# Constant waits in TensorE's loop, group work in single pieces, and weight loads put among tiles 3 to 11, in a fused attention, routing and expert kernel

## The reference

```python
scores = scale * np.matmul(q, k.transpose(0, 1, 3, 2))        # B = H = 8, S = 576, 64 per head
ret = scores * Dmat                                           # Dmat = gamma[h] ** (i - j) for i >= j, else 0
x = np.matmul(ret, v)                                         # then 4608 tokens x 512
logits = x @ phi                                              # 512 x 32 slots
d = exp(logits - logits.max(0)); d /= d.sum(0) + 1e-9         # over tokens
slot_input = d.T @ x                                          # 32 x 512
for e in range(8): slot_out[e] = np.maximum(slot_input[e] @ w1[e], 0) @ w2[e]
c = exp(logits - logits.max(1)); c /= c.sum(1) + 1e-9         # over slots
y = c @ slot_out
out = (((y @ fw1) * (y @ fw2)) @ w3) @ w_out
```

## Time and profile before

| | us |
|---|---|
| median of 3 runs (lowest, highest) | 422.67 (421.44, 427.01) |
| the profiled execution | 421.35 |
| its span, first to last instruction | 419.6 |
| TensorE busy | 359.9 (86% of the span), granted clock 0.972 |
| VectorE, GpSimd, ScalarE busy | 170.1, 162.5, 120.7 |
| DMA | 104.77 MB, 250 GB/s on average |

### The profile page before, as it was taken

How to read it: one execution, slowest core, us unless ns; L and a number is a source line. 1 busy time by engine, 2 the same in 40 slices (tenths; PEclk the granted TensorE clock), 3 DMA queues, 4 the chain that set the end, 5 groups by cost and what they waited for, 6 DMA issues and landing times. The chain is left out here.

```text
span 419.6 us, 16276 instructions
## 1 busy us (share of the span) xinstructions
PE 359.9 (86%) x7123; PEld 276.3 (66%) x7123; DVE 170.1 (41%) x353; ACT 120.7 (29%) x248; POOL 162.5 (39%) x155
## 2 busy tenths in 40 slices
PE   2568878878887788764999999989999999999996
PEld 1557766767576667652566655547878888888885
DVE  1334545655474466415400310069993223323220
ACT  1011121211121122122232523053264444454532
POOL 1520221122202122025435655139894555555530
PEclk9996999999898999986999999999999999999999
DMA  8557788888688779625799999705633555666322
GB/s 253 211 195 261 290 319 334 311 316 326 250 312 307 309 273 357 250 94 202 315 419 418 419 419 416 300 2 124 204 113 124 198 178 197 222 213 216 125 100 100
DMA packets 25914, 104.77 MB, mean 250 GB/s; under 512 B 2660, under 2 KB 5284, under 8 KB 16164
## 3 DMA queue, kind: packets, MB, share of 16 engines
q1 hardware_dynamic: 25892, 104.47, 66.8%
HBM read 94.14 MB, written 10.32 MB: 249 GB/s over the span
## 5 line engine op out<-in xcount | busy, mean ns | idle before, releaser
L546 POOL TENSOR_TENSOR pkg_sb<-pkg_sb,const_sb 128x512 f32<-128x512 f32 x36 | 37.7, 1048 | 128.6 <-DMA pkg_sb<-in_tiles 128.6
L602 POOL TENSOR_TENSOR feat<-c_sb 128x512 f32<-128x512 f32 x45 | 56.9, 1275 | 46.2 <-PE psum L999 44.3
L665 PE MATMUL psum<-weights_t,pkg_sb 64*64 64x64 f32 x1152 | 33.6, 232 | 31.8 <-issue 13.8
L999 PE MATMUL psum<-m_hi,feat_hi 128*128 128x512 f32 x144 | 56.1, 390 | 0.3 <-DVE m_lo L1453 0.3
L999 PE MATMUL psum<-m_lo,feat_hi 128*128 128x512 f32 x144 | 56.0, 389 | 0.0
L999 PE MATMUL psum<-m_hi,feat_lo 128*128 128x512 f32 x144 | 56.0, 389 | 0.0
L419 DVE TENSOR_TENSOR feat_lo<-feat,feat_hi 128x512 fp32r<-128x512 f32 x34 | 27.2, 800 | 62.2 <-ACT feat_hi L1140 61.0
L1015 ACT COPY x_nat<-psum 128x512 f32<-128x512 f32 x36 | 21.1, 585 | 108.2 <-PE psum L673 108.2
L1239 DVE TENSOR_TENSOR x_t<-psum,x_decay 128x512 f32<-128x512 f32 x36 | 24.9, 692 | 62.2 <-PE psum L665 62.2
L665 PEld LDWEIGHTS psum<-weights_t,pkg_sb 64*64 64x64 f32 x1152 | 26.3, 142 | 35.6 <-issue 35.5
L576 POOL TENSOR_TENSOR w_lo<-fold_raw,w_hi 128x512 fp32r<-128x512 f32 x16 | 21.1, 1321 | 51.8 <-ACT wo_hi L1073 51.7
(11 more groups left out here) (125 smaller groups left out, 565.0 us busy)
## 6 DMA issues: line engine op xcount, KB each, us to landing
pkg_sb<-in_tiles SPq DMA_DIRECT2D x34, 1024.0 KB, 4.9
unit_a<-in_units SPq DMA_DIRECT2D x16, 1024.0 KB, 12.2
c_sb<-c_rows SPq DMA_DIRECT2D x45, 256.0 KB
unit_x<-in_units SPq DMA_DIRECT2D x9, 1024.0 KB, 14.3
out<-out_sb SPq DMA_DIRECT2D x36, 256.0 KB, 2.1
fold_raw<-in_fold SPq DMA_DIRECT2D x6, 1024.0 KB, 7.1
unit_y<-in_units SPq DMA_DIRECT2D x5, 1024.0 KB, 12.5
unit_n<-in_units SPq DMA_DIRECT2D x4, 1024.0 KB, 13.7
```

What stands on the lines that cost most here:

```text
L546: nc.gpsimd.tensor_tensor(v_nat(n).rearrange("p (h d) -> p h d", h=HEADS), v_nat(n).rearrange("p (h d) -> p h d", h=HEADS), decay.unsqueez ...
L602: nc.gpsimd.tensor_tensor(feat[:, k, :], c_sb[:, s, x, :], c_sb[:, s, y, :], ALU.mult).then_inc(feat_ready, 1)
L665: last = mm(out_of(a, odd, half), v_nat(r)[rows, HD * h:HD * (h + 1)], weights_t[rows, r % 2, odd, HD * a:HD * (a + 1)], start=False, stop ...
L999: last = mm(psum[:, OUT + b, :], x, y, start=(at == 0 and m == 0), stop=(at == 4 and m == 2))
```

## The change

1. **Waits on constants.** TensorE lowers semaphores itself: `v_ready`, `states_ready`, `x_t_ready`, `logits_copied` and `phase_done` are counted down by a matmul that comes after the wait (`then_inc(..., -1)`), so each wait is for 1 (4 for `phase_done`) in every step. The wait for v of tile n+2, which stood before phase 1 of step n, stands before `scores` of step n+1. The wait for the states stands before the last four of the eight matmuls of phase 1. `masked`, `tile_begun`, and the waits for `x_nat_ready` in the loop are gone. The first scores now wait for v of tile 0 too. The dispatch of a group comes one step later.
2. **Group work in pieces.** DVE does one piece a step: `max_parts`, `max_slots`, `turn_exp`, `turn_raw`, `max_combine`, `shift_combine`, `sum_combine`, `divide_combine` at t = 0 to 7. The eight small copies of `max_logits` go to ACT (`move_parts` at t = 0, `spread_max` at t = 1).
3. **Loads.** SP issues two tiles ahead (2 and 3), then units 0 and 1, then after each tile from 4 to 11 one more megabyte: units 2 to 5, then the four pieces of `fold_raw`. Tiles 12 to 35 come with nothing between them.
4. **Three fold steps early.** ACT splits w = 0, 1, 2 at tiles 18, 22 and 26, POOL makes the low pieces at tiles 21 to 31. Their matmuls stay behind the loop, in the order 1, 5, 4, 2 parts instead of 2, 4, 4, 2. The places of w = 1 and 2 lie where the late fold pieces are loaded, so these loads now wait for `fold_used` 3.

```diff
@@ SP: loads
             load_first(1, 0)
+            load_first(1, 1)
             sp.dma_start(x_decay[:, :, 0:P], consts[:, C_XDECAY:C_ALL].rearrange("p (a n) -> p a n", a=PAIRS)
                          ).then_inc(decay_loaded, 16)
-            load_first(1, 1)
-            load_tile(2)
             sp.dma_start(const_sb[:, C_LATE:C_XDECAY], consts[:, C_LATE:C_XDECAY]).then_inc(const_late_loaded, 16)
             sp.dma_start(phi_sb[:, :, :], phi).then_inc(phi_loaded, 16)
-            weights = ([(load_first_unit, u) for u in range(6)]
-                       + [(load_fold, g, j) for g in (0, 2) for j in range(2)])
-            for n in range(3, NTILES):
+            load_tile(2)
+            load_tile(3)
+            load_first_unit(0)
+            load_first_unit(1)
+            for n in range(SLOTS_IN, NTILES):
                 load_tile(n)
-                if n >= 6 and n % 3 == 0:
-                    load, *which = weights[n // 3 - 2]
-                    load(*which)
+                if n < 2 * SLOTS_IN:
+                    load_first_unit(n - 2)
+                elif n < 3 * SLOTS_IN:
+                    load_fold(n // 2 % 2 * 2, n % 2)
...
                 if u in (12, 14):
+                    sp.wait_ge(fold_used, EARLY)
                     load_fold(1, u // 2 - 6)
@@ TensorE: counting down
+                            if (a, odd, half) == (0, 0, 0):
+                                last.then_inc(v_ready, -1)
...
+                            if half == 0 and (a, odd) == (0, 0):
+                                last.then_inc(states_ready, -1)
...
+                        if phase == 1 and (a, half) == (PAIRS - 2, 0):
+                            pe.wait_ge(states_ready, 1)
...
                             last.then_inc(phase_done if phase == 0 else out_ready, 1)
+                        elif phase == 1:
+                            last.then_inc(phase_done, -1)
...
+                    if a < 2:
+                        last.then_inc(x_t_ready if a == 0 else logits_copied, -1)
@@ TensorE: the step
+            def next_scores(r):
+                pe.wait_ge(v_ready, 1)
+                scores(r)
+                update(r)
+            def turn(r):
+                pe.wait_ge(logits_copied, 1)
+                pe.wait_ge(x_t_ready, 1)
+                turn_x(r)
...
-                    pe.wait_ge(x_t_ready, n)
-                    pe.wait_ge(x_nat_ready, n - 1 + NAT_AHEAD)
-                    pe.wait_ge(logits_copied, n - 1 + NAT_AHEAD)
-                    pe.sem_inc(tile_begun, 1)
-                    turn_x(before)
...
-                pe.wait_ge(phase_done, n * QUARTERS + QUARTERS)
-                if r < SLOTS_IN - 2:
-                    next_loaded(i, r)
-                    next_free(n)
-                    pe.sem_inc(tile_begun, 1)
...
+                pe.wait_ge(phase_done, QUARTERS)
                 through_scores(r, 1)
-            def next_loaded(i, r):
-                turn, place = divmod(r + 2, SLOTS_IN)
-                pe.wait_ge(tile_loaded[place], i * 16 + (turn + 1) * 16)
-                pe.wait_ge(v_ready, i * SLOTS_IN + (r + 3))
-            def next_free(n):
-                pe.wait_ge(masked, n + 2)
-                pe.wait_ge(states_ready, n * 2 + 5)
@@ TensorE: behind the loop
-            fold(2)
...
+            fold(1)
+            turn(SLOTS_IN - 1)
             logits(SLOTS_IN - 1)
-            fold(4)
+            fold(5)
             dispatch(GROUPS - 1)
             fold(4)
@@ ACT
+            def move_parts(g):
+                act.wait_ge(part_max, g + 1)
+                for j in range(SUBS):
+                    copy(neg_quad[:, j:j + 1], neg_part[SLOTS * j:SLOTS * (j + 1), :]).then_inc(parts_moved, 1)
+            def spread_max(g):
+                act.wait_ge(slot_max, g + 1)
+                for j in range(SUBS):
+                    copy(neg_max[SLOTS * j:SLOTS * (j + 1), g:g + 1], neg_slot[:, :]).then_inc(max_ready, 1)
...
                 if g > 0 and t == 0:
+                    move_parts(g - 1)
+                if g > 0 and t == 1:
+                    spread_max(g - 1)
                     exp_logits(g - 1)
-                if g > 0 and t == 4:
+                if g > 0 and t == 6:
                     exp_combine(g - 1)
+                if n in FOLD_HI_AT:
+                    split_hi(FOLD_HI_AT.index(n))
@@ POOL
+                if n in FOLD_LO_AT:
+                    w, second = divmod(FOLD_LO_AT.index(n), 2)
+                    fold_low(w, "wo" if second else "w3")
@@ DVE
                 if g > 0:
-                    if t == 0:
-                        max_logits(g - 1)
-                    if t == 2:
-                        shift_combine(g - 1)
-                    if t == 4:
-                        finish_combine(g - 1)
+                    for at, part in ((0, max_parts), (1, max_slots), (2, turn_exp), (3, turn_raw), (4, max_combine),
+                                     (5, shift_combine), (6, sum_combine), (7, divide_combine)):
+                        if t == at:
+                            part(g - 1)
```

More of the change, by code:

```diff
@@ L54 @@
 QUARTERS = 4
-NAT_AHEAD = 2
+EARLY = 3
+FOLD_HI_AT, FOLD_LO_AT = (18, 22, 26), (21, 23, 25, 27, 29, 31)
 C_MASK = 0
@@ L139, in build @@
         unit_f = place("unit_f", [P, 2, 2 * FF], at=fold_end - 48 * KB)
+        fold_early = [{n: place(f"{n}_early{i}", [P, D], F32R, at=fold_end - (32 - 8 * i - 2 * k) * KB)
+                       for k, n in enumerate(("w3_hi", "wo_hi", "w3_lo", "wo_lo"))} for i in range(2)]
         top[1] = fold_end - 32 * KB
@@ L1042, in copy_sums @@
                 copy(group_sum[:, g, :], psum[:, X_NAT, :]).then_inc(sums_copied, 1)
-            for done in (x_nat_ready, logits_copied):
-                act.sem_inc(done, NAT_AHEAD)
-            for n in range(NTILES):
-                g, t = divmod(n, TILES)
-                if n > 0:
-                    copy_x(n - 1)
-                    if g > 0 and n == dispatched_at(g - 1):
-                        copy_sums(g - 1)
-                    copy_logits(n - 1)
-                if g > 0 and t == 0:
-                    exp_logits(g - 1)
-                if g > 0 and t == 4:
-                    exp_combine(g - 1)
             def split_hi(w):
@@ L1092, in relu_hidden @@
                                          ACT.Relu).then_inc(hid_ready, 1)
+            act.sem_inc(logits_copied, 1)
+            for n in range(NTILES):
+                g, t = divmod(n, TILES)
+                if n > 0:
+                    copy_x(n - 1)
+                    if g > 0 and n == dispatched_at(g - 1):
+                        copy_sums(g - 1)
+                    copy_logits(n - 1)
+                if g > 0 and t == 0:
+                    move_parts(g - 1)
+                if g > 0 and t == 1:
+                    spread_max(g - 1)
+                    exp_logits(g - 1)
+                if g > 0 and t == 6:
+                    exp_combine(g - 1)
+                if n in FOLD_HI_AT:
+                    split_hi(FOLD_HI_AT.index(n))
             g = GROUPS - 1
-            split_hi(0)
             copy_x(NTILES - 1)
@@ L1325, in _ @@
             g = GROUPS - 1
-            max_logits(g)
+            max_parts(g)
+            dve.wait_ge(part_max, GROUPS)
+            for j in range(SUBS):
+                nc.vector.tensor_copy(neg_quad[:, j:j + 1], neg_part[SLOTS * j:SLOTS * (j + 1), :]).then_inc(parts_moved, 1)
+            max_slots(g)
+            dve.wait_ge(slot_max, GROUPS)
+            for j in range(SUBS):
+                nc.vector.tensor_copy(neg_max[SLOTS * j:SLOTS * (j + 1), g:g + 1], neg_slot[:, :]).then_inc(max_ready, 1)
             dve.wait_ge(max_ready, SUBS * GROUPS)
```

134 lines of the change are left out of this document (60 added, 74 removed).

## The result

The changed kernel takes 394.03 us (median of 4 runs, 393.1 to 394.45) where the kernel before takes 423.45 beside it on the same chip: a ratio of 0.929, 95% interval 0.923 to 0.936. The profiled execution has a span of 392.2 us where it was 419.6, so 27.4 us were won of the 33.2 forecast. The range held the time; the forecast of 389.5 was 4.5 us too low.

A forecast was written before the change was run, and what follows sets the result against it. TensorE's waits before the first expert unit bound the kernel, not the DMA; 21.9 us in the loop plus 11.3 behind it gave 33.2, a span of 386.4 and a median of 389.5 us, range 384 to 403.

The forecast's parts named there:

- Part 1: TensorE's waits in the loop: idle before phase 1 falls from 0.50 to 0.1 us, a step taking 3.39 us.
- Rival A: Loop step stays at 3.8 us, the 0.50 perhaps signal latency or colliding loads: 9.6 us, total 399; chance 0.17.
- Part 2: DVE's group work in the loop: 6.0 us of waits for states go; `sum_combine` costs 0.3 three times, 0.9 us.
- Part 4: Behind the loop: from its end to the first expert unit 13.2 us instead of 24.5, winning 11.3 us.
- Part 3: Loads in the loop: tile 4 lands at 24.5 us, tile 12 at 64.5, 16 megabytes in 40 us, queue never dry.
- rival C: Queue in the loop gives 340 GB/s, not 419: 16 megabytes take 49 us, total 398; chance 0.13.
- Rival B: Tiles 4 to 12 run at half clock while loads hold the loop: 4 to 7 us more, 395; chance 0.12.
- Rival D: Slower than before: code fetches behind full queue stop TensorE in first three passes, 7.3 us more each, 455; chance 0.04.
- Rival E: Counted waits pass a step late, so TensorE alternates with DVE; nothing won in the loop: 411; chance 0.03.

The follow-up runs named there:

- e_seq: Changed kernel with five increments of an unused semaphore put between TensorE's wait for phase 0 and phase 1: 411.99 us against 394.03.
- e_group: Changed kernel with DVE's group work back in lumps at t = 0, 2 and 4 and the copies on DVE: 403.28 us against 394.03.
- e_nofold: Changed kernel with no step of the fold prepared in attention, places, loads and TensorE's order kept: 406.43 us against 394.03.
- e_shift: Changed kernel with 48 more score matmuls, read by nobody, before the wait for v of tile 0: 397.59 us against 394.03.
- e_shift8: Changed kernel with the 48 extra score matmuls and the ten megabytes of weights behind tiles 8 to 17: 398.78 us against 394.03.
- e_from8: Changed kernel with the ten megabytes of weights behind tiles 8 to 17, one each, fold's first: 393.29 us against 394.03.
- e_third: Changed kernel with one megabyte of weights behind every third tile from 6 to 33, fold's first: 398.26 us against 394.03.
- e_half: Changed kernel with the weights in 20 pieces of 512 KB behind two of three tiles from 6 to 34: 393.16 us, ratio 0.930.

## Why the prediction was right, and where it was off

**Part 1** was right. "I take 0.1" for the wait that is left: 0.10. A step was to be 3.39 and is 3.44. Rival A (the 0.50 is the signal's latency) is out. e_seq shows that sequencer instructions between the wait and phase 1 bring the idle time back; how much of it is their number and how much that the wait no longer stands on the matmul, it does not show.

**Part 2** was right: no wait for states in the loop behind its first step. Even the 0.3 that I had left for `sum_combine` doesn't appear. e_group has the price of undoing it, 9.3 us by one run; part of it was never in the 6.0 of waits from which I worked.

**Part 4** was right in mechanism and size: 13.1 us for 13.2. In e_nofold the stretch is 11.1 longer, for the 11.3 forecast; the rest of its 12.4 is the loop that ends later.

**Part 3** held the step that failed: "I take 24.5 us for the landing of tile 4 again. Up to tile 12 the queue then has 16 megabytes: 40 us", with "so the queue does not run dry". The rate was right, even low: v of tile 7 to that of tile 12 is 24.4 us for ten megabytes, 430 GB/s, and rival C is out. But the queue is only as good as the places that TensorE frees, and I gave TensorE's first pass no stops of its own. They take 9.8 us. The first, 3.37, held back tile 0's place and so the load of tile 4, which I take for its 1.6; 3.88 and 1.49, with the 1.43 of slow matmuls, kept tile 2's place until 34.55. The DMA idled; over 12 to 60 us, in slices of 1.2:

```profile
GB/s 416 430 430 423 410 430 369 191 403 410 423 423 341 382 437 389 150 14 14 55 239 396 294 355 335 376 416 423 430 430 430 423 430 437 423 416 430 430 410 423
```

Four slices at 150, 14, 14 and 55, at 31 to 36 us, are most of the 6.0 us by which the loop ended late. That the stops are code is shown by e_shift, e_shift8 and the instruction packets. That a full queue makes them longer is clearest for the longest one: 3.88, 3.47 and 3.65 us in the three kernels with the changed order of the loads (changed, e_nofold, e_group), 1.53, 1.34 and 0.88 where no weights come before tile 6 (e_from8, e_third, e_half). The sum is less sure: 9.8, 7.9 and 7.9 in the same three, 6.8 to 7.0 in the other three. None of the four other packed or spread orders is worth anything that can be told: what they save in stops comes back as late v. So I know of no gain that the kernel left lying in its order; the miss is a cost that I had not counted.

**Rival B**, half clock in all the steps that the loads hold, did not come, but the half level did three times in the first 60 us. PE in the stretches 20:25 to 60:72 (busy us, granted clock, DMA share, GB/s):

```profile
20.00:25.00 5.00, 4.38 (x170) 0.83 0.93 347
25.00:30.00 5.00, 1.35 (x35) 0.85 1.02 400
30.00:35.00 5.00, 3.51 (x140) 0.80 0.34 136
35.00:40.00 5.00, 4.25 (x204) 1.00 0.79 262
40.00:50.00 10.00, 7.56 (x334) 0.95 0.98 404
50.00:60.00 10.00, 8.45 (x359) 0.88 1.01 425
60.00:72.00 12.00, 8.26 (x412) 1.00 0.99 419
```

Between 57 and 73 every step waits for v, 1.30 to 1.49 us of 4.9, at a granted clock of 1.00, the upper level (2.4 GHz). The lower level (1.2 GHz, a granted clock of 0.50) is there from about 18.3 to 21.7 us, from the end of the stop of 3.37 us on; from 28.5 to 32.0, from the end of the stop of 3.88 on; and from 49.0 to 52.4, behind the one wait for v of 2.21:

```profile
48.15 0.69 PE L645 MATMUL psum<-pkg_sb 64*64 64x64 f32 x32 [2.21 <-POOL pkg_sb L558]
48.63 0.82 PE L658 MATMUL psum<-pkg_sb 64*64 64x64 f32 x32
49.38 1.11 PE L700 MATMUL psum<-const_sb,x_t 128*128 128x128 f32 x4
```

The turns take 1.01 to 1.11 us in these three and 0.63 to 0.66 elsewhere. The third cost next to nothing, since the next v was ready only at 52.87; the second cost the 1.43 us above. Up to 15 us the runs take 1.10 to 1.13 us too, in both kernels and at a granted clock of 1.00; the profile does not show why. The Trainium skill (TensorE: Matmul & The Clock Gate, HAM oscillation) says that work in short pieces between DMA waits starts each piece at the low clock; this trace does not agree for waits of 1.3 to 1.5 us, and has one case for it at 2.2. e_nofold has one against it, a wait of 3.00 us at 49.48 with a granted clock of 1.00 behind it (49 to 53).

**Rival D** had the right mechanism and the wrong size. I priced a fetch behind a full queue at 7.3 us more; the longest stop was 3.88 in all, and the sum is 9.8 where it was 8.0 (5.4 and the 2.60 at 18.75). The Trainium skill (Runtime: NRT & Kernel Launch, Instruction fetch mechanics) says that an engine's code comes in 16 KB blocks over a DMA queue of its own, and that crossing from one to the next is mostly hidden. The trace agrees on the blocks (14 packets, 0.23 MB in the page's instruction queue, 15 and 0.25 in e_shift) and, in the first pass, not on the hiding: five of the six packets there go with a stop of 0.3 to 3.9 us. By its rule on taken branches D could have come in every pass; behind the first pass no stop is longer than 0.3 us, and from 43 us to the end of the loop no packet comes. The stop before phase 1 of step 0, which ends between 17.4 and 19.8 us in every kernel but the shifted ones, has its packet at 16.0 (14.9 to 16.6 in the others). Why the experts' new code shows no stop, with eight packets behind the loop, stays open.

**Rival E** is out with the steps of 3.44.

## What to carry to other kernels

When a loop's first pass feeds a ring of buffers, give TensorE's first run through new code stops of its own in the sum, some 7 us for this loop of four steps with a light queue and 8 to 10 with a full one, and what the clock adds behind a long stop (1.4 us here), and ask what the held buffers do to the loads; a rate of the queue is a forecast only as long as something frees its places. Before spreading background loads, compare the room of a single load (here 0.9 us) with the time of one piece (1.2 us for 512 KB): mean load says nothing while the piece is longer than the room. That is a condition and no guarantee: pieces of 0.6 us made tiles late as well. And count what stands on TensorE's sequencer between two runs of each step: five instructions there, with the wait ahead of them, were worth 18 us in 36 steps.

## What the runs showed of the hardware

- Five semaphore increments on TensorE's sequencer between a wait and the run behind it cost 0.61 us, 0.12 each (e_seq, with the wait no longer on the matmul).
- Increments by -1 on the matmuls add nothing that can be seen within a run: `scores` takes 0.68 before and after.
- In the first pass TensorE stops for 0.3 to 3.9 us inside runs of matmuls. 48 matmuls more ahead of them move the stops to other matmuls, and a lighter queue shortens them from 11.7 to 7.6 us, at the same matmuls (e_shift, e_shift8). In the four kernels compared each stop ends 2.2 to 2.8 us behind the start of a 16 KB packet of the instruction queue.
- Behind stops of 3.37 and 3.88 us and a wait of 2.21 the granted clock was 0.50 for about 3 us each (changed kernel); behind waits of 1.3 to 1.5 (changed kernel) and one of 3.00 (e_nofold) it stayed at 1.00.
- Loads of 1 MB in 8 KB rows follow each other in 2.44 us (430 GB/s) while TensorE, DVE and POOL all work.
